# Attention and two dense stages on one core: every large SBUF tensor moved to one offset modulo 512 bytes

## The reference

```python
q_assign = argmax(q_n @ c_n)          # nearest of 16 centroids of the head, unit vectors
k_assign = argmax(k_n @ c_n)
mask = q_assign[:, None] == k_assign[None, :]
scores = where(mask, (q @ k.T) / 8, -1e9)
attn = softmax(scores)
x = (attn @ v)                        # 1536 tokens x 512
h = (x @ w1) * (x @ w2) @ w3          # 512 -> 1024 -> 1024
y = h @ w_out                         # 1024 -> 512
h = y @ w_in                          # 512 -> 2048
g = maximum(h, 0) + alpha * minimum(h, 0)
out = g @ w_out2                      # 2048 -> 512
```

## The kernel before, in words

| tensors | before | after |
|---|---|---|
| `xh`, `xl`, `stage`, `ident`, `al` | 128 | 128 |
| `wc`, `q1` `k1` `q2` `k2`, `qk`, `vn`, `v12`, `ctab`, `cwin`, `ct`, `c16` | 192 | 128 |
| `oh` (behind the small `cmx`) | 288 | 224 |
| `early`, `pf`, `ph`, `pl`, `xo`, `rep`, `xf` | 416 | 128 |
| `w12`, `wcx`, `asb`, `ab`, `abh`, `abl` | 192 | 128 |
| `w34`, `gh`, `gl`, `neg`, `gf`, `ost` | 192 | 128 |

## Time and profile before

### The profile page before, as it was taken

How to read it: one execution, slowest core, us unless ns; L and a number is a source line. 1 busy time by engine, 2 the same in 40 slices (tenths; PEclk the granted TensorE clock), 3 DMA queues, 4 the chain that set the end, 5 groups by cost and what they waited for, 6 DMA issues and landing times.

```text
span 786.5 us, 10717 instructions
## 1 busy us (share of the span) xinstructions
PE 762.0 (97%) x3810; PEld 647.5 (82%) x3810; DVE 418.9 (53%) x636; ACT 329.3 (42%) x643; POOL 188.1 (24%) x210
## 2 busy tenths in 40 slices
PE   5999999999999998899999999999999999999998
PEld 4888998898899897788888888878888888888886
DVE  5335988989889886443211143276333443333332
ACT  4335978878888885532211142242112101020102
POOL 2131486876876873300000000000000000000000
PEclk9999999999999998999999999999999999999999
DMA  9645455554564322230000021232000000010001
GB/s 295 161 121 127 87 125 132 134 137 114 123 151 106 92 47 74 73 108 1 0 1 1 0 81 54 80 93 69 0 1 23 32 1 1 1 53 1 1 0 54
DMA packets 63579, 54.17 MB, mean 69 GB/s; under 512 B 31264, under 2 KB 51760, under 8 KB 63536
## 3 DMA queue, kind: packets, MB, share of 16 engines
q1 hardware_dynamic: 63536, 53.59, 26.4%
HBM read 31.50 MB, written 3.19 MB: 44 GB/s over the span
## 4 chain that ended last, share of the span: by engine, by line
PE 76%; POOL 15%; issue 5%; DVE 2%; ACT 2%; DMA 1%; POOLq 0%; SPq 0%; ACTq 0%
PE slot L580 55%; PE acc L580 17%; POOL xf L525 3%; PE slot L645 3%; POOL xf L521 2%; POOL xl L531 2%; POOL v L474 1%; POOL oh L500 1%; POOL v L470 1%; POOL c L492 1%; PE slot L693 1%; POOL c L493 1%; POOL c L498 1%; POOL c L490 1%; DMA early<-in_moe_w_out 1%
## 5 line engine op out<-in xcount | busy, mean ns | idle before, releaser
L580 PE MATMUL slot<-xh,w 128*128 128x512 f32 x768 | 252.7, 395 | 0.0
L580 PEld LDWEIGHTS slot<-xh,w 128*128 128x128 f32 x768 | 144.3, 188 | 34.9
L580 PE MATMUL slot<-xl,w 128*128 128x512 f32 x384 | 151.8, 395 | 0.0
L1049 ACT CAST gh<-gf 128x512 fp32r<-128x512 f32 x48 | 29.8, 621 | 207.8 <-PE acc L580 190.4
L1155 DVE TENSOR_TENSOR pl<-slot,ph 128x384 fp32r<-128x384 f32 x192 | 97.7, 549 | 14.0 <-ACT ph L919 13.8
L1149 DVE TENSOR_REDUCE nm<-slot 128x1 f32<-128x768 f32 x96 | 91.2, 950 | 21.4 <-PE slot L580 21.0
L919 ACT CAST ph<-slot 128x384 fp32r<-128x384 f32 x192 | 83.6, 487 | 40.4 <-PE slot L645 39.6
L911 ACT ACTIVATE pf<-slot,nm 128x768 f32<-128x768 f32 x96 | 87.9, 915 | 8.7 <-DVE nm L1149 8.5
L580 PEld LDWEIGHTS slot<-xl,w 128*128 128x128 f32 x384 | 72.2, 188 | 17.2
L645 PE MATMUL slot<-ident,pf 128*128 128x128 f32 x576 | 81.9, 277 | 1.9 <-DVE pl L1155 1.6
L580 PE MATMUL slot<-k,q 96*128 96x384 f32 (+1 forms) x384 | 83.6, 339 | 0.0
(11 more groups left out here) (117 smaller groups left out, 1084.5 us busy)
## 6 DMA issues: line engine op xcount, KB each, us to landing
stage<-in_moe_w SPq DMA_DIRECT2D x16, 256.0 KB, 3.2
stage<-in_moe_w_in SPq DMA_DIRECT2D x16, 256.0 KB, 2.7
stage<-in_moe_w_out SPq DMA_DIRECT2D x16, 256.0 KB, 3.0
stage<-in_moe_w SPq DMA_DIRECT2D x6, 512.0 KB, 4.2
qk<-in_q SPq DMA_DIRECT2D x16, 192.0 KB, 3.8
qk<-in_k SPq DMA_DIRECT2D x16, 192.0 KB, 4.2
vn<-in_v SPq DMA_DIRECT2D x16, 192.0 KB, 3.9
q<-k SPq DMA_DIRECT2D x16, 192.0 KB, 3.4
```

Of the source, the lines that this page charges most:

```text
L580: return nc.tensor.matmul(o, a, b, start=start, stop=stop)
L1049: copy(gh[j % 2][:, :], gf[j % 2][:, :]).then_inc(gh_done, 1)
```

## The change

`al` gets a row of 128 floats (512 bytes) of which 16 are used. `al16`, the raw form of alpha (16 x 128), has no tensor of its own any more: it is a view of `xf[1]`, which the attention uses later. `spare`, one of the small tensors, is widened by 288 bytes, so that the small tensors together fill a multiple of 512 bytes. No instruction is added or taken away, and no shape changes except the stated ones.

```diff
-        al = sb("al", [P, NJ])
-        al16 = sb("al16", [NJ, P])
+        al = sb("al", [P, P])
...
-        spare = sb("spare", [1, 2], F32, attn)
+        spare = sb("spare", [1, 74], F32, attn)
...
         xf = [sb(f"xf{i}", [P, 2, HS], F32, attn) for i in range(2)]
+        al16 = xf[1][0:NJ, 0, 0:P]
...
-            sp.dma_start(al16[:, :], alpha.rearrange("(j p) -> j p", p=P)).then_inc(ld_al, 16)
+            sp.dma_start(al16, alpha.rearrange("(j p) -> j p", p=P)).then_inc(ld_al, 16)
...
-                    nc.gpsimd.tensor_tensor(spare[0:1, :], zero[0:1, 0:2], zero[0:1, 0:2], ALU.add)
+                    nc.gpsimd.tensor_tensor(spare[0:1, 0:2], zero[0:1, 0:2], zero[0:1, 0:2], ALU.add)
...
-            nc.tensor.transpose(acc[:, 1, 0:NJ], al16[:, :], ident[0:NJ, 0:NJ]).then_inc(cen_turned, 1)
+            nc.tensor.transpose(acc[:, 1, 0:NJ], al16, ident[0:NJ, 0:NJ]).then_inc(cen_turned, 1)
...
-                copy(al[:, :], acc[:, 1, 0:NJ])
+                copy(al[:, 0:NJ], acc[:, 1, 0:NJ])
```

## The result

The changed kernel takes 777.23 us (median of 4, 776.43 to 778.21) against 787.27 us (median of 4, 786.77 to 788.28) for the kernel before. The ratio is 0.9871, 95% interval 0.9854 to 0.9888.

A forecast was written before the change was run, and what follows sets the result against it. TensorE alone was taken to bound the kernel after 326.4 us, with no single engine setting attention's time; 7.3 us plus 0.1 us off the 787.78 us median gave 780.4 us, range 778 to 785.

The forecast's parts named there:

- Layers 1 and 3, 1104 x 6.6 ns = 7.3 us: After 326.4 us, where TensorE alone sets the time, 1104 matmuls go from 233.3 to 226.7 ns, saving 7.3 us.
- The pair is: In layers 1 and 3, differing offsets of moving operand and weights, not either offset alone, set 233.3 instead of 226.7 ns.
- The detail of a collision with the weights loaded at the same time: At the last layer 3 matmul, its slow pace was said to fit streaming colliding with weights loaded for layer 4.
- If it is instead an after-effect of the unequal pair ... I take 0: First six matmuls of layer 2 and 4 groups: possible further gain of 1.4 us, counted as 0, kept for the range.
- readers of the banks: First six of layers 2 and 4: 1.38 instead of 1.36 us put down to VectorE and ScalarE reading banks just written.
- the 48 early matmuls: Layer 1 or 3 matmuls inside the last attention turn, before 326.4 us: gain 0 to 0.3 us, taken as 0.1.
- The base: Starting time for the whole kernel from which the 7.4 us gain was subtracted: the median, 787.78 us.
- The clock: Whole kernel: run to run spread allowed for by a few tenths of a us, on the upward side of the range.
- the forecast 452.8: Stretch from the first layer 2 matmul to the end: 452.8 us expected instead of 460.1.
- Attention, 0: Scores and product with v in attention: new offsets change nothing, taken as 0; at most 1.2 us gain.
- VectorE, ScalarE, GpSimd and transfers, 0: Other engines and loads: offsets change nothing, taken as 0; at most 0.7 us either way for engines, 1 us for a copy.
- The rule of two read ports: TensorE's separate SBUF ports for streaming operand and weights: the pair could not matter, 787.8 us; the rival standing for it got 0.10.

The follow-up runs named there:

- gap64: Changed kernel with a 64-byte gap behind `al`, giving layers 1 and 3 the unequal pair back; 787.0 us beside 786.59 us for the kernel before.
- gapff: Changed kernel with a 64-byte gap ahead of `w12` only, making layer 1 alone unequal; 782.32 us, ratio 0.994 to the kernel before.
- gapg: Changed kernel with `gh` and `gl` alone moved to 192, making layer 4 unequal; 783.33 us, ratio 0.995 to the kernel before.
- all192: Changed kernel with 64 bytes ahead of `xh`, so every large tensor lies at 192 modulo 512; 778.15 us, ratio 0.9888 to the kernel before.
- gatelate: Kernel before, with VectorE's alpha step of group j held until layer 4's group j-2 is done; 787.71 us, ratio 1.0015.
- accfirst: Kernel before, with layer 4's groups 0 to 14 doing the six `acc` matmuls before the six `slot` ones; 786.52 us, ratio 0.9993.
- nopad: Changed kernel without the 288 bytes in `spare`, leaving the small tensors unpadded; 777.82 us, ratio 0.9886 to the kernel before.
- gapph: Changed kernel with 64 bytes ahead of `pf`, making the 384-column product with v unequal; 778.09 us, ratio 0.9888 to the kernel before.
- gap224: Changed kernel with a 224-byte gap behind `al`, so weights of layers 1 and 3 lie 224 bytes from their moving operand; 788.11 us.

## Why the prediction was right in its mechanism and wrong in its size

- **Layers 1 and 3, 1104 x 6.6 ns = 7.3 us: right.** Both went from 233.3 to 226.7 ns. gap64, gapff and gapg give the cost back in all, in layer 1 alone, and move it to layer 4.
- **"The pair is" slow: right.** all192 excludes the offset itself, gapg excludes `xh` and `xl`. The detail of a collision with the weights loaded at the same time was wrong: the last matmul of layer 3 was slow for its own unequal pair, and is fast when only the weights loaded beside it lie apart (gapg).
- **"If it is instead an after-effect of the unequal pair ... I take 0": this step failed.** The term was 1.4 us (72 groups x 0.02) and was left out of the sum, because readers of the banks seemed to explain it. gatelate and accfirst show the after-effect. From the chains, 48 rounds of layers 3 and 4 gain 0.10 us each and the 22 rounds of layers 1 and 2 in the stretch 0.18 us each: 8.8 us, and with up to 0.3 for the 48 early matmuls 9.1, where the sum had 7.4. With 1.4 us more the forecast would have been 779.0, inside the range; the next two points took the time out of it.
- **The base.** The sum was taken from a median of three executions, 787.78 us. With one more it is 787.27, and beside the later experiments the kernel before had 786.4 to 786.9. That is 0.5 us of the miss in time, and nothing in the mechanism.
- **The clock: this term was too small.** About 1 us of the 10.0 us is left when 8.8 to 9.1 are taken off. At equal granted clock the difference is 8.7 to 9.0 us, and in the second comparison of the two kernels the medians differ by 9.3, the changed kernel's own being equal to 0.1 us in both. The rest thus most likely lies in which executions of the kernel before fell into the first comparison; their clocks, but for the profiled one's 0.993, are not known. The range had "a few tenths of run to run spread" for it, and upward only. That was too little, since the times at neighbouring values of the clock lie about 1 us apart in the kernel before, and one fall of the clock behind the wait costs 1.6. The last stretch of 449.3 us instead of the forecast 452.8 has the same two reasons, the after-effect and the clock, which stayed at 1.00 there.
- **Attention, 0: right.** Busy times agree to 0.5 us, and nopad and gapph find nothing beyond the spread. That 224 bytes are free held for 384 columns and does not for 512 (gap224: 7.00 us a round, the dearest).
- **VectorE, ScalarE, GpSimd and transfers, 0: right.** L1155 takes 549 ns before and after, and the loads of `q` and `v` land in 4.0 us each instead of 3.8 and 3.9, which nobody waits for.
- **The rule of two read ports.** The quoted section of the Trainium skill says that loading the next weights takes nothing from the running matmul. gapg agrees with that sentence as far as it goes: the last matmul of layer 3 starts its successor after 226 ns while weights 64 bytes apart are loaded. No run shows the ports. The step from there to "the pair could not matter" does not hold: 512-column matmuls whose weights lie 64 bytes beyond their moving operand cost 6.6 ns more each in every kernel here that has them.

## What to carry to other kernels

Where TensorE sets the time with 512-column float32r matmuls, compare start distances between groups of equal shape, not durations; a small constant excess in one group can be placement, which cost no instruction to mend here. Here it was enough that weights and moving operand of a matmul start at the same offset modulo 256 bytes, and one small tensor ahead of the large ones had broken that for 1152 matmuls. When two readings of a small excess fit the trace, do not set its price to nothing for the likelier one: give the sum under each, and test the readings on a group where only one of the two causes is present.

## What the runs showed of the hardware that was not expected

- A 512-column matmul whose weights lie 32, 64, 128 or 224 bytes (modulo 256) from its moving operand starts its successor about 6 to 8 ns later (6.97 to 7.00 us a round instead of 6.80; less 0.02 for the after-effect, over 24 matmuls). At 0 and 256 bytes there is no cost.
- At 448 bytes (64 short) a round of 30 takes 6.90 us, with a longer after-effect.
- The matmuls behind a group with 64 bytes between are slower too, though their own operands are equal: 1.38 instead of 1.36 us for six, in `slot` and in `acc` banks alike.
- The extra time goes with a matmul's own two operands: the last one before a group of unequal pairs starts its successor after 225 or 226 ns, the last one of such a group of layer 3 after 233.
- The same inequality costs nothing visible with 384 columns (174 and 175 ns).
- The granted clock fell to near half (0.50 to 0.60) for some 3 us behind a 2 us wait of TensorE in the profiled execution of the kernel before and in one of the two of the changed kernel, and stayed at 1.00 in the other, 1.6 us faster from there to the end.
